# Weight preparation and attention in one block with own buffers, and token places of the last block by comparison and product

## The reference

```python
# 1: attention with a feature map, q k v of (8, 8, 576, 64), w_phi of (64, 128)
proj = x @ w_phi;  proj = proj - max(abs(proj), axis=-1)
phi(x) = concatenate([exp(proj), exp(-proj)])
out = phi(q) @ (phi(k)^T v) / (phi(q) @ sum(phi(k)) + 1e-6)
# 2: a bilinear layer on the tokens x (4608, 512)
h = (x @ w1) * (x @ w2) @ w3;  x = h @ w_out
# 3: each token goes to the one expert of its largest logit
logits = x @ w_gate;  e = argmax(logits);  gate = softmax(logits)[e]
out[token] = gate * (relu(x @ w1[e]) @ w2[e])
```

## Time and profile before

| what | value |
|---|---|
| median of 3 runs | 1594.14 us (1583.5 to 1595.88) |
| profiled execution | 1591.94 us, span 1590.2 us |
| PE busy | 1514.4 us, 95% of the span |
| DVE, ACT, POOL busy | 835.1 (53%), 624.1 (39%), 447.8 us (28%) |
| clock granted to PE, mean | 0.977 of full speed |
| DMA | 134.93 MB, 85 GB/s over the span |

### The profile page before, as it was taken

How to read it: one execution, slowest core, us unless ns; L and a number is a source line. 1 busy time by engine, 2 the same in 40 slices (tenths; PEclk the granted TensorE clock), 3 DMA queues, 4 the chain that set the end, 5 groups by cost and what they waited for, 6 DMA issues and landing times.

```text
span 1590.2 us, 29388 instructions
## 1 busy us (share of the span) xinstructions
PE 1514.4 (95%) x8351; PEld 1313.6 (83%) x8352; DVE 835.1 (53%) x1614; ACT 624.1 (39%) x1333; POOL 447.8 (28%) x613
## 2 busy tenths in 40 slices
PE   5799999999899999999999999995999999999996
PEld 4699999999878888888888888774788888888885
DVE  3478888888735464654746547324333543332221
ACT  3378878888722122121121211232334443343221
POOL 1256666666810021020220202202122121212121
PEclk8899999999999999999999999997999999999998
DMA  5434444444430102021020220327333343211110
GB/s 192 144 89 110 104 109 104 108 108 106 126 123 0 63 18 79 0 79 61 18 79 0 79 66 13 92 74 172 119 115 124 142 155 130 105 36 40 43 46 22
DMA packets 84792, 134.93 MB, mean 85 GB/s; under 512 B 50144, under 2 KB 50400, under 8 KB 80530
## 3 DMA queue, kind: packets, MB, share of 16 engines
q1 hardware_dynamic: 76962, 114.01, 24.3%
q0 software_dynamic: 7792, 20.43, 3.8%
HBM read 104.52 MB, written 30.94 MB: 85 GB/s over the span
## 4 chain that ended last, share of the span: by engine, by line
PE 65%; DMA 2%; issue 2%; POOL 1%; DVE 1%; ACT 0%; DVEq 0%; POOLq 0%; ACTq 0%; SPq 0%
PE bank L156 61%; PE bank L1537 2%; DMA id_scratch<-rq,slot 1%; PE bank L1509 1%; DMA arena<-rows_scratch,ids 0%; POOL id_scratch L1006 0%; DMA arena<-rows_scratch,idg 0%; ACT big L802 0%; PE bank L1452 0%; DVE big L807 0%; DMA arena<-id_scratch 0%; PE bank L1460 0%; PE bank L1446 0%; POOL ids0f L1047 0%; POOLq L816 0%
## 5 line engine op out<-in xcount | busy, mean ns | idle before, releaser
L156 PE MATMUL bank<-big,xs 128*128 (+1 forms) x2112 | 507.4, 397 | 26.5 <-DVE xs L340 9.7
L156 PEld LDWEIGHTS bank<-big,xs 128*128 128x128 f32 x2112 | 395.0, 190 | 106.6 <-issue 17.3
L156 PE MATMUL bank<-xs,big 128*128 128x512 f32 x1728 | 397.2, 391 | 2.7 <-PEq L390 2.7
L156 PEld LDWEIGHTS bank<-xs,big 128*128 128x128 f32 x1728 | 324.8, 188 | 70.0 <-issue 2.9
L156 PE MATMUL bank<-big 128*128 128x512 f32 (+1 forms) x1632 | 327.4, 350 | 2.3 <-POOL big L465 1.4
L156 PEld LDWEIGHTS bank<-big 128*128 128x128 f32 (+1 forms) x1632 | 257.7, 166 | 37.1 <-POOL big L465 1.5
L1298 DVE TENSOR_TENSOR arena<-arena,bank 128x512 f32<-128x512 f32 x72 | 49.4, 686 | 245.2 <-PE bank L156 245.2
L1232 DVE CUSTOM_DVE_ANT_0 arena<-arena 128x512 f32<-128x512 f32 x256 | 159.4, 688 | 19.7 <-ACT arena L1123 19.7
L1000 POOL TENSOR_TENSOR arena<-arena 128x512 f32<-128x512 f32 x32 | 39.2, 1235 | 439.3 <-DMA arena<-rec_scratch 439.2
L1107 ACT COPY arena<-bank 128x512 f32<-128x512 f32 x72 | 42.3, 587 | 306.8 <-PE bank L156 306.8
L714 PE MATMUL bank<-v,arena 128*128 128x66 f32 (+1 forms) x1152 | 150.7, 273 | 6.3 <-DVE big L655 3.8
(11 more groups left out here) (145 smaller groups left out, 1312.6 us busy)
## 6 DMA issues: line engine op xcount, KB each, us to landing
arena<-we SPq DMA_DIRECT2D x32, 1024.0 KB, 4.9
kqraw<-kq SPq DMA_DIRECT2D x32, 576.0 KB, 3.7
rows_scratch<-arena SPq DMA_DIRECT2D x40, 256.5 KB
xT_scratch<-arena SPq DMA_DIRECT2D x32, 288.0 KB
v<-v SPq DMA_DIRECT2D x64, 128.0 KB, 2.4
arena<-xT_scratch SPq DMA_DIRECT2D x8, 1024.0 KB, 5.6
arena<-rec_scratch SPq DMA_DIRECT2D x64, 128.0 KB, 3.4
arena<-w3T SPq DMA_DIRECT2D x8, 512.0 KB, 4.2
```

The costliest lines, as they stand in the source:

```text
L156: ins = nc.tensor.matmul(out, left[a], right[b], start=first and n == 0, stop=last and n == 2)
```

## The change

It has five parts.

1. stage0 is gone. Its work stands ahead of the attention steps in stage1, in the same block. Seven of the eight w34 products come first, then project of the first pair, then the eighth product. mm_ps, the banks for w34, are now those of the numerators, so that the projections have their own.
2. Buffers: v, the w3 chunks, w_out and filler don't share bytes any more with what is loaded beside them, and w12st has two buffers. They lie in the bytes of kq's second pair, so the load of that pair waits for the last w12_low. w12_low moves from DVE to POOL.
3. The constants are written to HBM in the third and fourth step of attention.
4. x0 is loaded in two halves, and x0_high is cut in four casts, two in step c = 2 and two in c = 3, behind the exponentials of q.
5. Scattering and reading back of the last block's ids are gone. idrows is read before (blocks 0 to 7), DVE builds for each group q of 128 tokens two matrices by comparison (hotc: the column within a tile, 128x128; hotr: the tile, times token number, 128x288), and PE adds their products in PSUM to the transposed idrows (ids_by_place). The orders of PE, ACT, DVE, POOL and SP around it are rewritten: x_transpose(0) comes two products later, the ids products ahead of second_product(0), gather of tile 3 ahead of the first scatter, and SP loads the second expert's first three chunks only when the rows of the last block are written.

```diff
-        @block.sync
-            sp.wait_ge(wout_lo, WQ)
-            for u in range(2):
-                sp.dma_start(m["kqraw"][:, u], t["kq"][u]).then_inc(m["kq_in"][u], 16)
...
+            load_w3(2)
+            load_kq(0)
+            load_w12(0)
+            load_w3(3)
+            load_w12(1)
+            sp.wait_ge(masks_set, 2)
+            load_v(0, 0)
+            sp.dma_start(m["wgate"][:], t["w_gate"]).then_inc(small, 16)
+            for j in range(4, FC):
+                load_w3(j)
+                load_w12(j - 2)
+            load_v(0, 1)
+            for n in range(FC - 2, FC):
+                load_w12(n)
+            sp.wait_ge(w12_lo, FC)
+            load_kq(1)
...
+            def w12_low(n):
+                pool.wait_ge(w12_hi, n + 1)
+                pool.tensor_tensor(w12[:, 1, n], m["w12st"][n % 2], w12[:, 0, n].bitcast(F32),
+                                   ALU.subtract).then_inc(w12_lo, 1)
...
+            w12_low(0)
+            w12_low(1)
+            pool.wait_ge(kq_in[0], 16)
+            for g in range(NPG):
+                split_kq(pool, m, 0, 0, g)
+            for n in range(2, FC):
+                w12_low(n)
...
+            w3_high(1)
+            for j in range(OPEN):
+                w12_high(j)
+                if j + 2 < FC:
+                    w3_high(j + 2)
+                w34_high(j)
+            w12_high(FC - 1)
...
-                if at_end(b) and c == DC - 1:
-                    x0_high()
...
                 qexp(p, 0, not before(b, c, 1))
+                if at_end(b) and c >= 2:
+                    x0_high(2 * c - 4)
                 kexp(b, c, 4)
                 qexp(p, 1, not before(b, c, 1))
+                if at_end(b) and c >= 2:
+                    x0_high(2 * c - 3)
...
+            w3_low(1)
+            for j in range(OPEN):
+                if j + 2 < FC:
+                    w3_low(j + 2)
+                w34_low(j)
...
                 project(b, c, 3)
+                if not has1:
+                    for j in range(OPEN, FC):
+                        w34_product(j)
                 kv_products(b, c, 0)
...
-            load(CPE, 0)
             sp.wait_ge(ab_lo, FC * NB)
-            load(CPE + 1, 1)
             sp.wait_ge(rows_out, 16 * BQ * NB)
-            load(CPE + 2, 2)
+            for u in range(3):
+                load(CPE + u, u)
...
-            scatter_ids(NB - 1)
-            pool.dma_start(idrows, m["idtab"][0:3 * P * P, :].rearrange("(r p n) o -> p r (n o)", r=3, p=P)
-                           ).then_inc(idr_in, 16)
+            pool.wait_ge(idt_sb, 1)
+            pool.wait_ge(row_tab, 1)
+            pool.wait_ge(rows_out, 16 * BQ * NB)
+            gather(FIRST)
...
+            for q in range(BQ):
+                dve.tensor_scalar(hotc[:, q], m["colno"], col[:, q:q + 1], None, ALU.is_equal).then_inc(hot_done, 1)
+                dve.tensor_scalar(hotr[:, q], m["rowbase"], first_of[:, q:q + 1], token[:, q:q + 1],
+                                  ALU.is_equal, ALU.mult).then_inc(hot_done, 1)
...
+            def ids_by_place():
+
+                pe.wait_ge(slots_done, NB)
+                pe.wait_ge(idr_in, 16)
+                for r in range(3):
+                    pe.matmul(last_ps[:, r * P:(r + 1) * P], idrows[:, r], m["ident"][:],
+                              start=r == 0, stop=False, skip_group_check=True)
+                for q in range(BQ):
+                    pe.wait_ge(hot_done, 2 * q + 2)
+                    last = pe.matmul(last_ps[:, 0:E * TPE], hotc[:, q], hotr[:, q],
+                                     start=False, stop=q == BQ - 1, skip_group_check=True)
+                last.then_inc(idt_mm, 1)
```

More of the change, by code:

```diff
@@ new lines, in _ @@
+            load_w3(0)
+            for h in range(WQ):
+                sp.dma_start(wout[:, h * KQ:(h + 1) * KQ],
+                             t["w_out"].rearrange("p (k n) -> p k n", k=FC)[:, h * KQ:(h + 1) * KQ]
+                             ).then_inc(wout_in[h], 16)
+            load_w3(1)
+            sp.wait_ge(cst, 3)
+            for half in range(2):
+                sp.dma_start(m["wphi"][half * D:(half + 1) * D, half * DF:(half + 1) * DF], t["w_phi"]
+                             ).then_inc(wphi_in, 16)
@@ L527, in _ @@
             pairs(sp, step)
+            sp.wait_ge(small, 16)
             store(LAST, DC - 2)
@@ L770, in step, with w34_product @@
                 transposes(b, c, 1)
+            def w34_product(j):
+                pe.wait_ge(w3_lo, j + 1)
+                if j >= 2:
+                    pe.wait_ge(w34_lo, j - 1)
+                for k in range(FC):
+                    if j == 0 and k % KQ == 0:
+                        pe.wait_ge(wout_lo, k // KQ + 1)
+                    last = split3(nc, mm_ps[j % 2][:], parts(w3s[:, :, j % 2, k, :]), parts(wouts[:, :, k, :]),
+                                  k == 0, k == FC - 1)
+                last.then_inc(w34_mm, 1)
+            for j in range(OPEN):
+                w34_product(j)
             pairs(pe, step)
@@ L1119, in turn @@
                 for q in range(BQ):
+                    if not more and q >= 1:
+                        turned(q - 1)
+                    if not more and q == 2:
+                        rows_high(0)
                     act.wait_ge(x2_mm, BQ * i + q + 1)
@@ L1517, in first_product @@
                 for c in range(DC):
+                    if c == DC // 2 and between is not None:
+                        between()
                     last = split3(nc, h_ps[h][:], parts(xt[:, :, c]),
@@ L1562, in _ @@
             pe.matmul(x2T_ps[:, 0:E], m["ones"][:], m["cum"][:, BQ * E:], start=True, stop=True).then_inc(cnt_mm, 1)
-            first_product(1, 1, 0, 0)
+            h_transpose(0)
+            for h in range(2):
+                first_product(1, h, 0, 0)
             x_transpose(2)
+            ids_by_place()
             second_product(0, 0, 0)
@@ L1569, in _ @@
                 first_product(2, h, 0, 0)
+            x_transpose(3)
             second_product(1, 0, 0)
[L1571 to L1575 removed]
             h_transpose(2)
[L1577 removed]
+            pe.wait_ge(tabs, 2)
+            pe.wait_ge(row_tab, 1)
             last_tile = tiles(pe, tile)
```

478 lines of the change are left out of this document (223 added, 255 removed).

## The result

| | before | after |
|---|---|---|
| median | 1595.01 us (4 runs, 1583.5 to 1598.99) | 1535.12 us (4 runs, 1533.38 to 1537.55) |
| ratio | | 0.9634, 95% interval 0.9589 to 0.9679 |
| profiled execution | 1591.94 us | 1533.38 us |
| mean granted clock | 0.977 | 0.997 |

The kernel became 60 us faster, 3.7%; forecast were 1536. The profiled executions differ by 58.56 us, forecast were 56.0. In a later group of runs the kernel before took 1583.32 us (9 runs) and the changed one 1535.73 (5 runs), a ratio of 0.9695 (0.9682 to 0.9708). The smaller gain belongs to the kernel before, which has two levels: all nine of these runs are at 1582 to 1587, while most others are at 1589 to 1599.

A forecast was written before the change was run, and what follows sets the result against it. PE was busy for 95% of the span, so only its idle time and low-clock stretches could be won. Gains of 25.3, 6.2 and 24.5 us sum to 56.0, taking the profiled 1591.94 to 1535.9, forecast 1536 us; range 1522 to 1556.

The forecast's parts named there:

- Opening: From the start to the second pair's first projection: that projection at 61.7 instead of 87.0, 25.3 us gained.
- collision of DVE and POOL: In the opening, subtracts from SBUF on both engines share ports: product 2 starts at 21.8 instead of 20.6.
- The cover: In the opening, the second kq is ready at 58.7, 3.0 us before PE needs it.
- End of attention: PE's stop of 3.78 us and the low clock behind it go: net 6.2 us gained, bounds 3 and 8.
- no stop above 1 us in the last sequence: Sign that the forecast holds, to be seen in PE's timeline after the change.
- Junction: Last block to first tiles: 31.6 us of stops and low clock lost before, less new costs, 24.5 us gained.
- The fourth tile's gather: In the junction, 11.8 us of gather chain beside 11.9 of PE work; 1.5 us charged for slower gathers.
- The loop's entry: Entering the loop of tiles, PE reads three table words too: 2.0 us charged, bounds 0 and 4.
- The thin cover: Rival, 26%: late weight loads in junction and opening stop ACT and PE and drop the clock; 16 us worse, 1552.
- The clock falls in the short stops too: Rival, 7%: remaining stops of 1.3, 1.6 and 2.0 us each cost up to 2.5 us more; 1543.
- No change: Rival, 1%: both of PE's long gaps come back in other places; 1590.
- slower: Rival, 2%: the weights' stream governs the loop of tiles, PE waiting 2 us in each of 37 tiles; 1610.

The follow-up runs named there:

- low_on_dve: The changed kernel with DVE instead of POOL doing the subtracts of the w12 chunks in the opening; 1534.34 us.
- after_again: The changed kernel run once more, unedited; 1535.73 us.
- eight_first: The changed kernel with the opening's eighth 512-column product ahead of the first pair's projection instead of inside it; 1540.59 us.
- end_as_before: The changed kernel with the end of attention as before: x0 loaded in one portion, POOL's first scaling one piece earlier, four casts together; 1540.94 us.
- cast_together: The changed kernel with ACT's four casts of x0 together again, behind all of POOL's scaling; 1535.48 us.
- ids_by_memory: The changed kernel with the last block's ids going by memory again (scatters, read back, three transposes) and the orders tied to that; 1555.77 us.
- wide_arena: The kernel before with only the arena of buffers enlarged, 12840 instead of 12802 words a partition; a single run, 1586.04 us.
- tiles_only: The kernel before's opening, attention and buffers with the changed kernel's stage2 (junction and loop of tiles); 1566.53 us, ratio 0.9832 to the kernel before.

## Why the prediction was right

**What bounds the kernel.** Right: nearly all of the gain was PE's idle time (47.2 us less) and the low clock behind it (11.4 us less of busy time).

**Opening, 25.3 forecast, 26.2 measured.** The collision of DVE and POOL came as forecast (2.58 us; low_on_dve shows its cause), but hid itself, since product 1 ended at about 21.2, not 20.5, and the data came 1 us earlier. project took 2.9 for 2.8 (48.19 to 51.07), and the eighth product 5.5. The second kq was issued at 52.44 and POOL had it at 57.80, 5.4 us instead of the 3.7 of the earlier trace rows; its first group was split at 59.01, and PE used it at 60.86. The cover was 1.9 us instead of 3.0; it held. The 0.9 between forecast and measured says little: the same opening reaches the second projection at 61.95 in after_again's profile, a gain of 25.1. eight_first shows what the eighth product covers.

**End of attention, 6.2 forecast, 6.4 measured;** 4.9 by after_again's profile, 5.2 by end_as_before's median. The size was right. The mechanism was too narrow: the term named the casts, and cast_together shows that they alone don't bring it back. The new stop before POOL's last subtract was forecast at 1.2 and is 1.38; the prediction's sign "no stop above 1 us in the last sequence" contradicts its own term here.

**Junction, 24.5 forecast, 28.1 measured.** Here two terms were mis-sized, both on the careful side. The fourth tile's gather cost 0 instead of 1.5: the rows table was done at 1042.4, POOL issued at 1044.50, and PE came at 1050.34. The loop's entry cost nothing (0.84 us between the last h_transpose and the loop's first product, 0.79 within the loop) instead of 2.0. The others hit: rows_low 1.56 for 1.6, the ids products 2.4 for 2.0. ids_by_memory shows that of the 28 some 20 hang on the way of the ids and the orders tied to it.

**Not in the sum.** The loop of tiles lost 1.8 us with the arena's size. The prediction named a tile slower than 12.2 us as a sign of trouble; it was 12.30 after 12.25, for a reason that it didn't think of.

**The rivals.** The thin cover held in every profile of the changed kernel, though not for want of a sign: ACT did wait 3.22 us for weights ahead of h_high(1), which the prediction had named as a sign of being wrong. It cost nothing, as ACT then still waited 2.57 us for PE. With the scatters back (ids_by_memory) the same wait is 11.11 us and reaches PE, so the prediction's argument against this rival, that the scatter is gone, was the right one. "The clock falls in the short stops too", at 7%, was forecast as all or nothing. It is true of a part of the executions, and likely a source of the kernel's scatter of 3 to 4 us. "No change" and "slower" had no sign.

**The kernel before.** The prediction took the stop of 5.87 us as fixed. It is one of two cases, and in the group of runs at the lower level the change is worth 47.6 us. Had the profile before shown the other case, the forecast gain and the measured one would both be some 7 us smaller (the 7.7 us of wide_arena), and the forecast time the same.

## What to carry to other kernels

A chain through memory with 4-byte scatters is paid in latency, 13 to 19 us here beside 1 MB loads, and it delays these loads too; 2.4 us of extra products on the engine that bounds are cheap against it. When a stop is taken for fixed, look whether two engines reach a shared resource within a few tenths of a microsecond of each other: order, not work, then decides 5 us, and moving the consumer is safer than tuning the producer. Price a short stop of PE at its length plus a chance of a fall of the clock (here five of eight, 1.3 to 2.0 us), and take the last short ones away together.

## What the runs showed of the hardware

- POOL's issue of the first gather took 1.01 to 1.02 us when it began ahead of a DVE subtract of 128x2048 from SBUF (six profiles), and 2.41 to 3.11 when it began 0.08 to 0.78 us behind one (eight profiles); it then ended 0.9 us after that subtract.
- The granted clock behind one and the same stop of PE differs between executions: 1.00 in three and 0.50 in five profiles behind 1.36 to 1.38 us, 1.00 in seven and 0.50 in two behind 1.56. tiles_only kept 1.00 behind 2.62 us, by its 6 matmuls of 288 columns in 1.01 us, wide_arena behind the 2.66 between the stages, and ids_by_memory behind 3.58, by its 24 matmuls of 512 columns in 5.70 us.
- In wide_arena, where the landings are in the trace, the last block of 4-byte scatters landed 11.8 us after the end of its last issue, beside weight loads (1070.92 to 1082.67); that of the block before it took 6.1 (1012.05 to 1018.15).
- 38 words more per partition in front of the small buffers made the first product of a tile, 24 matmuls, take 5.58 us instead of 5.54, with the same instructions.
